# Scores and values on quarters of the array, odd heads with swapped token halves, and another order of a unit

## What is computed

```python
for t in range(S):                                    # r, k, v: (B, H, S, D) = (4, 8, 768, 48)
    kt, vt, rt = (k[:, :, t], v[:, :, t], r[:, :, t])
    cur = np.einsum('bhd,bhe->bhde', u[None] * kt, vt)
    y[:, :, t] = np.einsum('bhd,bhde->bhe', rt, state + cur)
    state = w[None, :, :, None] * state + np.einsum('bhd,bhe->bhde', kt, vt)
x = y.transpose(0, 2, 1, 3).reshape(B * S, H * D)     # 3072 x 384
logits = x @ phi                                      # 32 slots
slot_input = softmax(logits, 0).T @ x                 # 4 slots for each of 8 experts
slot_out = relu(slot_input @ w1[e]) @ w2[e]
x = softmax(logits, 1) @ slot_out
h = x @ w_in
out = where(h > 0, h, exp(min(h, 0)) - 1) @ w_out
```

## Time and profile before

| | |
|---|---|
| median of 3 plain runs | 401.15 us (399.9 to 401.28) |
| the profiled execution | 404.44 us |
| its span | 402.7 us |
| PE busy in the span | 391.3 us, 97% |
| DVE, ACT, POOL busy | 268.0, 220.0, 103.4 us |
| granted clock, mean of the span | 0.987 |

### The profile page before, as it was taken

How to read it: one execution, slowest core, us unless ns; L and a number is a source line. 1 busy time by engine, 2 the same in 40 slices (tenths; PEclk the granted TensorE clock), 3 DMA queues, 4 the chain that set the end, 5 groups by cost and what they waited for, 6 DMA issues and landing times.

```text
span 402.7 us, 9822 instructions
## 1 busy us (share of the span) xinstructions
PE 391.3 (97%) x3597; PEld 344.4 (86%) x3597; DVE 268.0 (67%) x514; ACT 220.0 (55%) x496; POOL 103.4 (26%) x132
## 2 busy tenths in 40 slices
PE   8799999999999999999999999999999999999997
PEld 6698888888876335469999999999999999999996
DVE  5567777777766731199976677677667667767771
ACT  1587767676766104168746446544644564455441
POOL 5676767676750000055510000000000000000000
PEclk9799999999999899999999999999999999999999
DMA  6899999999999979941002000100200020002002
GB/s 125 191 225 231 216 237 224 234 230 226 230 278 334 419 281 405 405 130 37 2 0 81 0 2 9 69 0 0 78 0 0 0 78 0 0 0 80 1 1 80
DMA packets 87469, 51.74 MB, mean 128 GB/s; under 512 B 76944, under 2 KB 82192, under 8 KB 86416
## 3 DMA queue, kind: packets, MB, share of 16 engines
q1 hardware_dynamic: 87440, 51.38, 44.7%
HBM read 45.86 MB, written 4.72 MB: 126 GB/s over the span
## 4 chain that ended last, share of the span: by engine, by line
PE 88%; DVE 4%; DMA 3%; issue 2%; ACT 2%; POOL 1%; SPq 0%; DVEq 0%; POOLq 0%; ACTq 0%
PE psum L914 16%; PE psum L916 16%; PE psum L915 16%; PE psum L594 6%; PE psum L850 5%; PE psum L627 5%; PE psum L563 5%; PE psum L762 3%; PE psum L635 3%; PE psum L607 3%; DMA w<-in_moe_w_dram 3%; PE psum L642 2%; PE psum L618 1%; PE psum L781 1%; ACT scores L1208 1%
## 5 line engine op out<-in xcount | busy, mean ns | idle before, releaser
L916 PE MATMUL psum<-w_out_hi,elu_lo 128*128 128x384 f32 x372 | 125.8, 338 | 0.0
L914 PE MATMUL psum<-w_out_hi,elu_hi 128*128 128x384 f32 x372 | 125.7, 338 | 0.0
L915 PE MATMUL psum<-w_out_lo,elu_hi 128*128 128x384 f32 x372 | 125.3, 337 | 0.0
L1317 ACT ACTIVATE exp_h<-psum 128x512 f32<-128x512 f32 x96 | 57.7, 601 | 100.5 <-PE psum L850 100.4
L1174 DVE SCALAR_TENSOR_TENSOR elu<-psum,neg_part 128x512 f32<-128x512 f32 x96 | 66.2, 690 | 57.1 <-ACT neg_part L1304 57.1
L915 PEld LDWEIGHTS psum<-w_out_lo,elu_hi 128*128 128x128 f32 x372 | 69.8, 188 | 3.8
L914 PEld LDWEIGHTS psum<-w_out_hi,elu_hi 128*128 128x128 f32 x372 | 70.4, 189 | 0.0
L916 PEld LDWEIGHTS psum<-w_out_hi,elu_lo 128*128 128x128 f32 x372 | 69.9, 188 | 0.0
L1166 DVE TENSOR_TENSOR elu_lo<-elu,elu_hi 128x512 fp32r<-128x512 f32 x96 | 67.1, 699 | 0.6
L1304 ACT ACTIVATE neg_part<-exp_h 128x512 f32<-128x512 f32 x96 | 59.9, 626 | 1.7 <-DVE elu L1174 1.4
L1208 ACT ACTIVATE scores<-ident,bonus 128x128 f32<-128x128 f32 x192 | 58.7, 390 | 3.2 <-DVE bonus L957 3.2
(11 more groups left out here) (155 smaller groups left out, 415.1 us busy)
## 6 DMA issues: line engine op xcount, KB each, us to landing
w_sb<-in_moe_w_dram SPq DMA_DIRECT2D x24, 512.0 KB, 4.9
...
```

The lines of the kernel that those rows point to most:

```text
L914: pe.matmul(acc, hi, w_out_hi[:, f, :], start=(f == 0), stop=False)
L915: pe.matmul(acc, hi, w_out_lo[:, f, :], start=False, stop=False)
L916: m = pe.matmul(acc, lo, w_out_hi[:, f, :], start=False, stop=(f == KF2 - 1))
L1317: act.activation(exp_h[:, f % 2, :], banks[4 + f % RING][:, :], ACT.Exp).then_inc(exp_done, 1)
```

## The change

- **Quarters.** `attend` and `values` work on quarters of the array (64 x 64) and leave the masked quarter out: 16 matmuls each, 8 over 128 columns and 8 over the last 64. `values` comes in two parts, so that the row tiles write to different banks at any time; a new semaphore `y_half_done` stands between them.
- **Odd heads** (`rev`) are held with their token halves swapped (tokens 64 to 127 in rows 0 to 63). r, k, v and u are laid out as even heads, then odd heads; the transposes of r for odd heads go through a swapped identity; mask, diagonals and the key table follow.
- **Loads.** One load call takes two batches, as three DMAs (even heads; each half of the odd heads). The first k goes through ACT's queue. w1 comes in other pieces: 1 MB in chunk 0, 2 MB in chunks 1 to 4, 3 MB in the last.
- **Order.** On PE a unit is now: key_values, turn_k and turn_r of the next unit, turn_x, logits, state_in, values part 0, attend of the next unit, values part 1. On DVE r_to_sbuf comes first and bonus last; on ACT y_to_sbuf, k_to_sbuf, diagonals of the unit after next.
- **Start.** The first matmuls fill 4 x 128 columns in banks 2 and 3 (were 2 x 128); the two warming matmuls before unit 0 go.

```diff
-        ident = place("ident", [P, P], F32)
+        ident_wide = place("ident_wide", [P, P + HP], F32)
+        ident, ident_swap = ident_wide[:, 0:P], ident_wide[:, HP:HP + P]
...
-        r_raw = place("r_raw", [P, B, H, HP], F32)
-        k_raw = place("k_raw", [P, B, H, D], F32)
-        u_row = place("u_row", [P, H, D], F32)
+        r_raw = place("r_raw", [P, 2, B, H // 2, HP], F32)
+        k_raw = place("k_raw", [P, 2, B, H // 2, D], F32)
+        u_row = place("u_row", [P, 2, H // 2, D], F32)
...
-                sp.dma_start(w1_sb[:, n, :], w1_dram[n // KD][:, n % KD, :]).then_inc(w1_loaded, 16)
+            def load(out, x, c, g, loaded):
+                bs, t0 = slice(2 * g, 2 * g + 2), c * P
+                even, odd = (x[rev, bs].rearrange("b t i d -> t b i d") for rev in range(2))
+                sp.dma_start(out[:, 0, bs, :, 0:D], even[t0:t0 + P]).then_inc(loaded[g], 16)
+                sp.dma_start(out[0:HP, 1, bs, :, 0:D], odd[t0 + HP:t0 + P]).then_inc(loaded[g], 16)
+                sp.dma_start(out[HP:P, 1, bs, :, 0:D], odd[t0:t0 + HP]).then_inc(loaded[g], 16)
...
-                for b in range(B):
-                    un = c * B + b
+                for g in range(2):
+                    un = c * B + 2 * g
+                    if un > 0 and not (last and g == 1):
+                        sp.wait_ge(y_done, un)
+                        load_v(c + g, 1 - g)
                     if not last:
-                        load_w1(un)
-                    elif b == 0:
-                        for n in range(un, E * KD):
-                            load_w1(n)
-                    if not last:
-                        sp.wait_ge(bonus_ready, un + 1)
-                        sp.wait_ge(k_scaled, max(un + 1, 2))
-                        sp.wait_ge(r_turned, un + 1)
-                        sp.wait_ge(k_turned, un + 1)
-                        load_r(c + 1, b)
-                        load_k(c + 1, b)
-                    if not (last and b >= 1):
-                        wait_for(sp, y_done, un)
-                        load_v(c + (b + B - 1) // B, (b + B - 1) % B)
+                        sp.wait_ge(bonus_ready, un + 2)
+                        sp.wait_ge(k_scaled, un + 2)
+                        sp.wait_ge(k_turned, un + 2)
+                        load_k(c + 1, g)
+                        sp.wait_ge(r_turned, un + 2)
+                        load_r(c + 1, g)
+                    if first:
+                        load_w1([g], slice(2, KD))
+                    elif not last:
+                        load_w1([2 * (c - 1) + g], slice(0, 2))
+                    elif g == 0:
+                        load_w1(range(2, E), slice(2, KD))
...
             load_r(0, 0)
-            load_k(0, 0)
-            sp.dma_start(u_row[:, :, :].rearrange("p h d -> p (h d)"), u_flat.broadcast_to([P, DM])
-                         ).then_inc(u_loaded, 16)
+            for rev in range(2):
+                sp.dma_start(u_row[:, rev], u_sets[rev].broadcast_to([P, H // 2, D])).then_inc(u_loaded, 16)
+            load_v(0, 0)
             load_r(0, 1)
             load_k(0, 1)
-            load_v(0, 0)
-            for b in range(2, B):
-                load_r(0, b)
-                load_k(0, b)
-                load_v(0, b - 1)
+            load_v(0, 1)
...
+            for i, n in ((2, 4), (3, 4), (6, 2), (5, 2)):
+                pe.matmul(banks[i][:, 0:n * P].rearrange("p (n t) -> p n t", n=n), ones[:, :],
+                          ones[:, :].unsqueeze(1).broadcast_to([P, n, P]), start=True, stop=True)
+            def turn(turned, nat, last_pairs):
                 for a in range(PAIRS):
-                    m = pe.transpose(turned[:, a * P:(a + 1) * P], nat[:, 2 * a:2 * a + 2, :], ident[:, :])
+                    m = pe.transpose(turned[:, a * P:(a + 1) * P], nat(a), ident if a < 2 else last_pairs)
                 return m
+            def r_pair_raw(b):
+                return lambda a: r_raw[:, a // 2, b, 2 * (a % 2):2 * (a % 2) + 2, :]
             def turn_r(un, b, c):
-                pe.wait_ge(r_loaded[b], 16 * (c + 1))
+                pe.wait_ge(r_loaded[b // 2], LOADED * (c + 1))
                 wait_for(pe, r_ready, un)
-                turn(banks[0], r_raw[:, b]).then_inc(r_turned, 1)
+                turn(banks[0], r_pair_raw(b), ident_swap).then_inc(r_turned, 1)
...
                 pe.wait_ge(r_ready, un + 1)
                 pe.wait_ge(k_ready, un + 1)
                 wait_for(pe, scores_ready, 2 * un)
-                for a in range(PAIRS):
-                    for two in range(2):
-                        rows = slice(two * HP, two * HP + D)
-                        m = pe.matmul(ps_A[two][:, a, :], k_pair[rows, i, a, :], r_pair[rows, i, a, :],
-                                      start=True, stop=True)
+                pe.nop(nofuse=True)
+                for cols, first in ((slice(0, P), 0), (slice(HP, P), 1)):
+                    for n in range(2):
+                        for two in range(2):
+                            for half, a in ((0, n + 2 * first), (1, n + 2 - 2 * first)):
+                                rows, e0 = slice(two * HP, two * HP + D), half * HP
+                                m = pe.matmul(ps_A[two][e0:e0 + HP, a, cols], k_pair[rows, i, a, e0:e0 + HP],
+                                              r_pair[rows, i, a, cols], start=True, stop=True, skip_group_check=True)
                 m.then_inc(A_done, 1)
...
-            def values(un, b, i, first):
-                pe.wait_ge(scores_ready, 2 * un + 2)
-                for two in range(2):
-                    for a in range(PAIRS):
-                        h, e0 = 2 * a + two, (a % 2) * HP
-                        m = pe.matmul(ps_y[e0:e0 + HP, two, (a // 2) * P:(a // 2) * P + P], v_sb[:, b, h, :],
-                                      scores[:, i, h, :], start=(first and a < 2), stop=(a >= 2), skip_group_check=True)
-                m.then_inc(y_done, 1)
+            def values(un, b, i, first, part):
+                if part == 0:
+                    pe.wait_ge(scores_ready, 2 * un + 2)
+                else:
+                    pe.wait_ge(y_half_done, un + 1)
+                pe.nop(nofuse=True)
+                for q_is_half, cols in ((True, slice(0, P)), (False, slice(HP, P))):
+                    for half in range(2):
+                        two = half if part == 0 else 1 - half
+                        q = half if q_is_half else 1 - half
+                        for e in range(2):
+                            h, rows = 2 * (2 * q + e) + two, slice(half * HP, half * HP + HP)
+                            m = pe.matmul(ps_y[e * HP:e * HP + HP, two, q * P + cols.start:q * P + P],
+                                          v_sb[rows, q, b, 2 * e + two, :], scores[rows, i, h, cols],
+                                          start=(first and part == 0 and q_is_half),
+                                          stop=(part == 1 and not q_is_half), skip_group_check=True)
+                m.then_inc(y_half_done if part == 0 else y_done, 1)
...
             def attend_chunk(c, first, last):
                 for b in range(B):
                     un, i = c * B + b, b % 2
-                    if first and b == 0:
-                        keep_clock_up(2)
                     if not last:
                         if not first and b == 1:
                             pe.wait_ge(lT_ready, c)
                         if not first and b == 2:
                             pe.wait_ge(logits_ready, c)
                         key_values(un, b, i, c, 2 if first and b == 0 else un + 1)
-                    if not (last and b == B - 1):
-                        attend(un + 1, 1 - i)
+                    if not (first and b == 0) and not (last and b == B - 1):
+                        turn_k(un + 1, 1 - i, un + 2)
+                        turn_r(un + 1, (b + 1) % B, c + (b + 1) // B)
                     if last and b == B - 1:
                         turn_exponentials()
-                    if not first:
-                        state_in(un, b, i, c)
-                    if first and b == 1:
-                        pe.wait_ge(r_ready, 2)
-                    if not (first and b == 0):
+                    elif not (first and b == 0):
                         turn_x(un - 1, (b - 1) % B)
                     if not first and b == 0:
                         pe.wait_ge(phi_loaded, 64)
                         if not last:
                             pe.wait_ge(state_summed, un + 1)
                         chunk_logits(c - 1)
-                    if not (last and b >= 2):
-                        turn_r(un + 2, (b + 2) % B, c + (b + 2) // B)
-                        turn_k(un + 2, i, un + 3)
+                    if not first:
+                        state_in(un, b, i, c)
                     if last:
-                        pe.wait_ge(v_loaded[b], 16 * CHUNKS)
-                    values(un, b, i, first)
```

(77 more changed lines are left out.)

161 lines of the change are left out of this document (93 added, 68 removed).

## The result

| | before | after |
|---|---|---|
| median of 20 runs, us | 400.99 | 403.85 |
| lowest and highest | 399.9 to 403.1, and one of 541.4 | 400.4 to 409.0 |
| profiled execution, us (span) | 404.44 (402.7) | 400.42 (398.4) |

The ratio is 1.0049, 95% interval 1.0027 to 1.0071: 0.5% slower, where 3.1% faster was forecast (388.5 us, range 384 to 397). The profiled execution of after is its fastest one, that of before is slower than its median, so the two profiles set side by side show a gain that the medians do not.

The account below looks back on a forecast made before the run. PE was taken to bound attention, with the DVE-ACT ring (3.94 us a unit) taking over. Start and chunk 0 -1.7, four middle chunks -8.8, last chunk -2.2: -12.7 from 401.15 gives 388.5 us, range 384 to 397.

Parts of the forecast that it names:

- Slots: PE's matmuls: records on different tiles run side by side; a slot costs 0.105 us at 128 columns, 0.060 at 64.
- rival 1: PE's attend and values: 64-column matmuls get no cheaper, PE's unit 4.13 us, total 392; chance 0.14.
- cold row: First matmuls at the start, 64 columns on the low clock: 8 slots at 0.107 us, thus about 0.055 warm.
- Rings: DVE and ACT waiting on each other: a lap of 3.94 us a unit, 0.05 above PE's 3.89.
- Rivals 2, 5 and 6: 2: DVE/ACT waits make units 4.2 us, 0.15; 5: four tiles overlap only by two, 0.04; 6: bound untouched, excluded.
- The prediction's own test: Whole kernel: the prediction is wrong if the middle chunks do not give two thirds of the gain.
- Scores and values by quarters: PE's unit: attend 0.66 us (was 1.09), values two parts of 0.33 (was 1.02), unit 3.89, 0.64 less.
- about 5 of 8.5 us, covered: SyncE's queue: issuing nine DMAs a half chunk besides w1 takes about 5 of 8.5 us, so costs nothing.
- rival 3: Middle chunks: the DMA holds them at 18.5 to 19.4 us, only the ends gain, total 395.5; chance 0.15.
- Start: Up to unit 0's key_values: +1.0 us (bounds 0 and +2.5); with chunk 0's -2.7, together -1.7.
- rival 4: First chunk: the clock stays low, three more units at half speed, +9 us, total 397.5; chance 0.05.

Follow-up runs that it names:

- after_again: The changed kernel, unchanged, run and traced a second time; ratio 1.0015 (0.9982 to 1.0048) to the kernel before.
- no_loop_loads: The changed kernel without the loads of r, k and v for chunks 1 to 5 (output not the reference's); median 394.63 us.
- odd_one_dma: The changed kernel with odd heads loaded by one DMA, halves not swapped (output not the reference's); chunk 3 took 17.14 us.
- w1_late: The changed kernel with all 12 MB of w1 loaded from the last chunk on; chunk 3 took 17.14 us.
- k_by_sp: The changed kernel with the first load of k issued by SyncE behind that of r, instead of on ScalarE's queue; 403.90 us.
- before_again: The kernel before, unchanged, run and traced a second time; 402.03 us, ratio 1.0004 (0.9981 to 1.0028).

## Why the prediction was wrong

By its steps, on the profiled execution (forecast for after 391.7; measured 400.42, and 402.41 in after_again):

```
                                     forecast   after   after_again
up to unit 0's key_values              14.7     15.4     15.0
chunk 0                                16.3     15.2     16.5
chunk 1 (19.8 - 2.2)                   17.6     21.6     20.2
chunk 2                                17.2     17.1     17.1
chunk 3                                17.2     18.3     18.6
chunk 4 and last chunk (36.5 - 4.4)    32.1     34.8     36.6
up to the first expert matmul           9.9     11.6     12.4
up to the first w_out matmul           37.3     36.7     36.5
```

- **Slots and PE's unit: right to 0.02 us.** attend 0.67 (0.66), values 0.34 and 0.33 (0.33 each), unit 3.89. That matmul records get cheaper with 64 columns (rival 1) was the disputed point, and the cold row told it rightly. The Trainium skill ("TensorE: Matmul & The Clock Gate", section "Wait — 56ns, not 53.3ns?") has start-to-start never below about 25 ns. The trace differs: 32 records of `attend` in 0.67 us are 21 ns each, half of them with 128 columns. So the figure does not hold for records spread over four tiles; whether it holds for one tile no run here shows.
- **Rings and chunks: right where nothing disturbs them.** 17.0 to 17.14 in chunks 2 and 3 of no_loop_loads, odd_one_dma and w1_late, forecast 17.2. Rivals 2, 5 and 6 fall with it. The prediction's own test, two thirds of the gain in the middle chunks, fails: chunk 2 gains 2.3 us, chunk 1 loses 0.4 to 1.8.
- **The step that failed, missing: the arrival of PE's own instructions.** The sum priced every record ("Slots", "Scores and values by quarters") and put the bringing of the code at nothing without a word; so the 2.2 us a middle chunk, 8.8 in all, and the 2.2 of the last were taken whole. The earlier trace rows shows 688 records in 19.39 us, the new kernel has 932 in 17.14, and no step asked who brings them. Most of the excess of chunk 1 (+4.0 and +2.6), part of that of the last chunk, and the wait at `chunk_logits_T` ahead of the experts come from it: 3.7 to 7.4 us in an execution, and 1.6 more for a stretch of low clock behind one. The two traces of one kernel differ in these waits, which probably is why after spreads over 8.6 us and before, its one outlier aside, over 3.2; no other execution was traced. No rival stood for this; the range ended at 397 for lack of it.
- **Mis-sized: SyncE's issue.** "about 5 of 8.5 us, covered" took 0.37 and 0.58 of the earlier trace rows for the new DMAs. In chunks 2 to 4 most took 0.37 to 0.9, v's last up to 1.5, and k's first in each half chunk 2.3 to 3.1; a half chunk took 8.6 to 10.0 us in sum, as long as PE's half chunk or longer. In w1_late, where w1's 1 MB does not stand ahead of them, none takes over 0.76 in chunks 2 to 4: SyncE is held by what drains ahead of it. That is rival 3 in mild form: 18.3 to 18.6 for chunk 3, and the last chunk's r late. That the issue is full is shown; that it is what lengthens a chunk is not, since k_by_sp has it nearly as full (8.1 to 9.3) at 17.14.
- **Start: +1.3 to +1.7 where +1.0 was taken**, inside its bounds (all traces with this start lie at 14.1 to 15.4, those of the old one at 12.9 to 14.1). The first matmuls took 4.50 (3.78 before, 1.9 more was reckoned); the delay runs through the table of decays instead. Chunk 0 gained 2.5 to 3.8 (forecast 2.7); rival 4 did not come. The 3.8 is partly luck: after was on the low clock for 3.41 us there, before and after_again for 6.83.
- **The base.** before's profiled run lay 3.3 us over the median, and the prediction took its -12.7 over from the one to the other. before_again's lay 2.1 over, after_again's on its median. The runs of before made beside the other kernels go with the granted clock: those with a mean of 0.987, as both its profiled ones have, had a median of 402.8 us, those at 0.991 400.8, those at 1.000 399.7. So the profile was an execution with more low clock than most, and a gain reckoned on its low stretch (chunk 0's 2.3) is not to be had in full by the median. Of the 14.0 us between 388.5 and after_again's 402.45, 10.7 are the steps of the table (402.41 - 391.7) and 3.3 are this base.
- **The chances.** The cases that end below 399.1 us add up to 0.96, where "faster than 399.1" has 0.91.

In no_loop_loads, which lacks the loads, the profiled 396.45 less its waits (4.6 with the small ones) and 1.6 for the low clock is 390.3, and 391.7 was forecast for the profiled execution. That is a sum and no run, but it says that instructions and loads together are enough for the miss in the profile's terms.
